# One slot sooner for key grams and norm, eight slots from 12 for the inverse's steps, and a small weight product in four parts

## What is computed

```python
for t in range(S):                                   # per batch and head: delta-rule attention
    y[:, :, t] = q[t] @ state
    state = state + beta[t] * outer(k_n[t], v[t] - k_n[t] @ state)   # k_n: k over its norm
x  = y.transpose(0, 2, 1, 3).reshape(3072, 384)
h  = x @ w_in
x2 = maximum(0.01 * h, h) @ w_out
logits = x2 @ w_gate + modality_bias[modality_id]
e = argmax(logits); gate = softmax(logits)[e]
out = gate * (maximum(x2 @ w1[e], 0) @ w2[e])        # one expert for each token
```

## Time and profile before

| what | us |
|---|---|
| median of 3 runs | 1021.66 (1021.15 to 1023.77) |
| the profiled execution's own time | 1023.64 |
| its span, first to last instruction | 1021.9 |
| PE busy (matmuls) | 932.1, 91% of the span |
| DVE busy | 554.3, 54% |
| ACT busy | 351.7, 34% |
| POOL busy | 87.8, 9% |
| mean granted clock of PE | 0.951 of full speed |

### The profile page before, as it was taken

One profiled execution on the slowest core, in us unless ns is written; L12 is line 12 of the kernel. 1 busy time (PEld: TensorE's weight loads), 2 busy tenths in 40 slices (PEclk: granted clock), 3 DMA queues, 4 the chain that ended last, 5 costly groups with the idle time before them and its releaser, 6 DMA issues.

```text
span 1021.9 us, 26857 instructions
## 1 busy us (share of the span) xinstructions
PE 932.1 (91%) x10524; PEld 832.1 (81%) x10525; DVE 554.3 (54%) x1577; ACT 351.7 (34%) x608; POOL 87.8 (9%) x100
## 2 busy tenths in 40 slices
PE   4897699999999999999999999999988999999972
PEld 4896588878888889888888888888877898888962
DVE  5936795389626983498428862334562333333341
ACT  4255234542534343433444242332511222212230
POOL 1000000000020000100010001001021212212211
PEclk8659899999999999999999999999998999999996
DMA  9803181235223440345143411317132111111122
GB/s 161 283 2 73 36 159 57 72 87 88 56 47 89 95 80 26 87 103 94 26 87 81 86 30 29 98 38 202 40 112 99 46 31 46 38 39 46 31 78 70
DMA packets 147923, 77.91 MB, mean 76 GB/s; under 512 B 112112, under 2 KB 143856, under 8 KB 147440
## 3 DMA queue, kind: packets, MB, share of 16 engines
q1 hardware_dynamic: 143728, 66.98, 27.9%
q0 software_dynamic: 4096, 9.48, 3.0%
HBM read 59.30 MB, written 13.21 MB: 71 GB/s over the span
## 4 chain that ended last, share of the span: by engine, by line
PE 73%; DVE 12%; DMA 4%; ACT 3%; issue 3%; SPq 3%; DVEq 0%; POOL 0%; ACTq 0%; POOLq 0%
PE bank L486 16%; PE bank L471 14%; PE bank L567 10%; PE bank L542 9%; PE bank L430 3%; PE bank L457 2%; PE bank L415 2%; PE bank L454 2%; PE bank L362 2%; SPq L737 2%; PE bank L552 2%; DVE inv_t L1264 2%; DVE inv_tmp L1258 2%; PE bank L504 2%; PE bank L383 1%
## 5 line engine op out<-in xcount | busy, mean ns | idle before, releaser
L486 PE MATMUL bank<-wo_hi,g_hi 128*128 128x392 f32 x384 | 138.8, 361 | 8.3 <-DVE g_lo L1338 5.4
L1011 ACT ACTIVATE g_raw<-bank 128x512 f32<-128x512 f32 x96 | 57.3, 597 | 227.4 <-PE bank L471 225.0
L1333 DVE SCALAR_TENSOR_TENSOR g_raw<-g_raw 128x512 f32<-128x512 f32 x96 | 66.2, 690 | 123.6 <-ACT g_raw L1011 122.8
L471 PE MATMUL bank<-x_hi,wi_hi 128*128 128x512 f32 x288 | 118.2, 411 | 16.1 <-DVE x_lo L1329 12.6
L486 PE MATMUL bank<-wo_hi,g_lo 128*128 128x392 f32 x384 | 132.0, 344 | 0.0
L486 PE MATMUL bank<-wo_lo,g_hi 128*128 128x392 f32 x384 | 131.8, 343 | 0.0
L471 PE MATMUL bank<-x_hi,wi_lo 128*128 128x512 f32 x288 | 113.7, 395 | 0.0
L471 PE MATMUL bank<-x_lo,wi_hi 128*128 128x512 f32 x288 | 113.6, 394 | 0.0
L1018 ACT ACTIVATE g_hi<-g_raw 128x512 fp32r<-128x512 f32 x96 | 60.6, 631 | 105.7 <-DVE g_raw L1333 102.6
L1338 DVE TENSOR_TENSOR g_lo<-g_raw,g_hi 128x512 fp32r<-128x512 f32 x96 | 66.1, 689 | 41.8 <-ACT g_hi L1018 40.9
L486 PEld LDWEIGHTS bank<-wo_hi,g_hi 128*128 128x128 f32 x384 | 72.7, 189 | 14.2 <-issue 6.8
(11 more groups left out here) (211 smaller groups left out, 1664.2 us busy)
## 6 DMA issues: line engine op xcount, KB each, us to landing
wo_lo<-wo_lo_d SPq DMA_DIRECT2D x80, 196.0 KB
w_raw<-in_moe_w SPq DMA_DIRECT2D x6, 1536.0 KB, 8.4
x_rows<-stage SPq DMA_DIRECT2D x6, 770.0 KB
kq_in_rows<-in_k SPq DMA_DIRECT2D x6, 768.0 KB, 5.4
k_raw<-in_k SPq DMA_DIRECT2D x24, 192.0 KB, 4.6
vals<-in_v SPq DMA_DIRECT2D x24, 192.0 KB, 4.7
kq_in_rows<-in_q SPq DMA_DIRECT2D x6, 768.0 KB, 7.8
x_raw<-y_t SPq DMA_DIRECT2D x36, 96.0 KB, 2.5
```

The costliest lines, as they stand in the source:

```text
L471: mm = pe.matmul(bank[0][:], a[:, m, P * f:P * f + P], x[:, m, :], start=(m == 0 and x is x_hi and a is wi_hi), stop=(m == KT - 1 and a is ...
L486: mm = pe.matmul(acc[i][:, 0:DX], g[f % 2][:, P * i:P * i + P], w, start=(f == 0 and k == 0), stop=(f == FT - 1 and k == 2))
L1011: act.activation(g_raw[f % 2][:], bank[0][:], ACT.Copy).then_inc(s.hs_ev, 1)
L1333: dve.scalar_tensor_tensor(out=g_raw[f % 2][:], in0=g_raw[f % 2][:], scalar=0.01, in1=g_raw[f % 2][:], op0=ALU.mult, op1=ALU.max).then_inc ...
```

## The change

The table gives the steps of the inverse to eight slots from 12 on, where it gave them to eight from 13 on. The key grams (`gram_k`, their copies, `norm`, `roots`, `scale_gram`) stand a slot sooner in every set, and all four `keys_t` in slot 8. `gate_weights` is cut at slices 9, 11 and 14: nine slices stay in slot (-1, 4), two go to slot 11, three to slot 12 between the two parts of `state_sum`, two to slot 13 ahead of `up(0, 0)`. The tiles `wo_t` move off x_raw to a place that `no_token` also holds, so ACT waits for the end of `clear_list`'s transfer ahead of its first copy; SP's wait ahead of `load_x(0)` goes.

```diff
-INV_AT = {13: (0, 5), 14: (5, 9), 15: (9, 13), 0: (13, 17), 1: (17, 21), 2: (21, 25), 3: (25, 30), 4: (30, INV)}
+INV_AT = {12: (0, 4), 13: (4, 8), 14: (8, 11), 15: (11, 15), 0: (15, 19), 1: (19, 23), 2: (23, 27), 3: (27, INV)}
...
-        wo_t = [same_place(f"wo_t{i}", [P, KT, P], sb.at + 4 * DM * i, F32) for i in range(2)]
+        wo_t = [same_place(f"wo_t{i}", [P, KT, P], sb.at + at, F32) for i, at in enumerate((2560, 6144))]
...                                       # PE
+                    gate_weights(14, FT)
                     up(0, 0)
...
-                    if f == 10:
-                        gram_k(n + 2, 0)
-                    if f == 11:
-                        gram_k(n + 2, 2)
...
                 if n == -1 and f == 4:
-                    gate_weights()
+                    gate_weights(0, 9)
+                if n == -1 and f == 11:
+                    gate_weights(9, 11)
+                if n == -1 and f == 12:
+                    gate_weights(11, 14)
...
                     if f == 8:
-                        keys_t(n + 2, 0)
-                        keys_t(n + 2, 1)
+                        for m in range(4):
+                            keys_t(n + 2, m)
                     if f == 9:
-                        keys_t(n + 2, 2)
-                        keys_t(n + 2, 3)
+                        gram_k(n + 2, 0)
+                        gram_k(n + 2, 1)
                     if f == 10:
-                        gram_k(n + 2, 1)
-                    if f == 11:
+                        gram_k(n + 2, 2)
                         gram_k(n + 2, 3)
...                                       # SP
-                if n == -1 and f == 10:
-                    sp.wait_ge(s.wx_mm, FT)
...                                       # ACT
+            def gate_weights(first, end):
+                if first == 0:
+                    act.wait_ge(s.list_out, 16)
+                for f in range(first, end):
...
-                    if f == 12:
                         roots(n + 2)
...
+                if n == -1 and f == 11:
+                    gate_weights(9, 11)
                 if n == -1 and f == 12:
+                    gate_weights(11, 14)
                     split_x(0)
...                                       # DVE
-                if nxt and f == 13:
+                if nxt and f == 12:
                     scale_gram(n + 2)
...
-                    if f == 12:
                         norm(n + 2)
```

More of the change, by code:

```diff
@@ L488, in down @@
                 mm.then_inc(s.l2_mm, 1)
[L490 to L493, removed]
+            def gate_weights(first, end):
+                if first == 0:
+                    pe.wait_ge(s.misc_in, 16 * 6)
+                for f in range(first, end + 1):
+                    if f < end:
                         if f % 4 == 0:
@@ L500, in gate_weights @@
                         mm.then_inc(s.wt_mm, 1)
-                    if f:
+                    if f > first:
                         pe.wait_ge(s.wt_ev, f)
@@ L1025, in copy_acc, with gate_weights @@
                     act.activation(stage[:, i, :], acc[i][:, 0:DX], ACT.Copy).then_inc(s.acc_ev, 1)
-            def gate_weights():
-                for f in range(FT):
+            def gate_weights(first, end):
+                if first == 0:
+                    act.wait_ge(s.list_out, 16)
+                for f in range(first, end):
                     act.wait_ge(s.wt_mm, f + 1)
@@ L1032, in gate_weights, with gate_columns @@
                     act.activation(wo_t[f % 2][:].rearrange("p a b -> p (a b)"), bank[2 + f % 3][:, 0:DM], ACT.Copy).then_inc(s.wt_ev, 1)
+            def gate_columns():
                 act.wait_ge(s.wx_mm, FT)
@@ L1062, in slot @@
                 if n == -1 and f == 13:
+                    gate_weights(14, FT)
+                    gate_columns()
                     small_h(0, 0)
@@ L1102, in slot @@
                     if f == 8:
-                        copy_t(k_t, "KT", n + 2, 0)
-                        copy_t(k_t, "KT", n + 2, 1)
+                        for m in range(4):
+                            copy_t(k_t, "KT", n + 2, m)
                     if f == 9:
-                        copy_t(k_t, "KT", n + 2, 2)
-                        copy_t(k_t, "KT", n + 2, 3)
+                        copy_gram(n + 2, 0)
                     if f == 10:
-                        copy_gram(n + 2, 0)
+                        copy_gram(n + 2, 2)
                     if f == 11:
-                        copy_gram(n + 2, 2)
-                    if f == 12:
                         roots(n + 2)
@@ L1506, in slot @@
                     split_x(0)
+                    rest_gate_weights()
                     leaky(0, 0)
                     rest_g(0, 0)
-                inv = range(*INV_AT[f]) if f in INV_AT and (nxt if f >= 13 else cur) else range(0)
-                inv_set = n + 2 if f >= 13 else n + 1
-                if nxt and f == 13:
+                inv = range(*INV_AT[f]) if f in INV_AT and (nxt if f >= 12 else cur) else range(0)
+                inv_set = n + 2 if f >= 12 else n + 1
+                if nxt and f == 12:
                     scale_gram(n + 2)
@@ L1540, in slot @@
                 if nxt:
+                    if f == 9:
+                        copy_gram(n + 2, 1)
                     if f == 10:
-                        copy_gram(n + 2, 1)
+                        copy_gram(n + 2, 3)
                     if f == 11:
-                        copy_gram(n + 2, 3)
-                    if f == 12:
                         norm(n + 2)
@@ L1561, in slot @@
                 if n == -1 and f == 5:
-                    rest_gate_weights()
                     token_biases()
```

## The result

The changed kernel took 1025.66 us (median; 1024.03 to 1027.08), the kernel before on the same chip 1021.66. The ratio is 1.0045 with an interval of 1.0023 to 1.0066: slower by 4.6 us (the medians are 4.0 apart), where 1.1 less was forecast. The median is 1.4 above the upper end of the range. The profiled execution took 1025.3, with a span of 1023.5. That is only 1.6 above the span before; the rest of the difference does not show between these two traces.

The account below looks back on a forecast made before the run. It took the small product, then DVE's chain, to bound the ramp, and PE the rest; 4.0 us later at `up(0, 0)` less 1.5, 0.8, 1.2 and 1.6 gave -1.1, so 1021.66 became 1020.6 us, range 1014.0 to 1024.3.

Parts of the forecast that it names:

- Step 1: Slot (-1, 4): ACT's first copy waits for the list until 43.3, `merge_x` starts at 59.3, 5.6 us sooner; 4.5 taken as gained.
- Steps 2 and 3: Ramp, slots 8 to 13: norm's transpose one us sooner, product slices delay `up(0, 0)` by 8.5 us, 4.0 net, to 110.3.
- Steps 4 to 6: Behind `up(0, 0)`: -1.5 at `split_wo(0)`, -0.8 at `tr`, -1.2 at x_lo of block 1, -1.6 at `tr` in four other blocks.
- The sum of -1.1: Whole kernel: 4.0 - 1.5 - 0.8 - 1.2 - 1.6 = -1.1 us, span 1021.9 to 1020.8.
- step 6: Sets 2 to 5: shorter waits of `merge_x` for `tr`, 4 x 0.4 = -1.6 us; moved pieces in slots 8 to 13 cost nothing.
- rival 3: Slots 8 to 10: bunched transposes and grams wait for banks, four sets x 0.5, +2.0 us, 1022.6; chance 0.14.
- the prediction's own signs of being wrong: `up(0, 0)` starting before 107 or after 112.5, or new PE waits in slots 8 to 10 of blocks 0 to 3.
- Rival 1: Slots 11 to 13 of the ramp: product slices run at full clock, 6.4 us less, 1014.2; chance 0.22.
- rival 2: Behind `up(0, 0)`: clock stays low through `down(0, 0)` and `up(0, 2)`, +4.2 us, 1024.8; chance 0.12.
- Rival 4: Slot (-1, 4): list lands at 48.9 us or later, so the 4.5 us are lost, 1025.1; chance 0.04.

Follow-up runs that it names:

- no_list: Changed kernel with `wo_t` where `no_token` does not reach, so ACT's first copy does not wait for `clear_list`'s transfer; 1012.69 us, ratio 0.9957 to the kernel before.
- copy_ahead: Changed kernel with ACT's copies of slices 9 and 10 put ahead of `roots` in slot 11; 1014.63 us, ratio 0.9934 to the kernel before.
- rest_behind: Changed kernel with slices 9 to 15 of the product in one piece in slot 13, behind both halves of `state_sum`; 1018.13 us, ratio 0.9999 to the kernel before.
- gate_alone2: Kernel before with only the product in four parts and `wo_t` moved, run once more; 1026.74 us, ratio 1.0069, no pauses.
- before_trace3: Kernel before, unchanged, third trace; `up(0, 0)` at 105.9 us, no pauses.
- after_third: Changed kernel, unaltered, run a third time on another chip; 1019.73 us, ratio 0.9988 to the kernel before, no pauses.
- after_fourth: Changed kernel, unaltered, run a fourth time; 1021.64 us, ratio 0.9998 to the kernel before, no pauses.
- set 2: Kernels measured together on another chip: the kernel before (1019.35 us), no_list, rest_behind, and the changed kernel with key grams singly (1019.02 us).
- before_trace4: Kernel before, unchanged, fourth trace; `up(0, 0)` at 103.1 us, two small pauses.
- grams_alone: Kernel before with only grams and norm a slot sooner and the table from 12; 1026.2 us, ratio 1.0049; once more in a set without pauses: 1020.1 us, 1.0003.
- gate_alone: Kernel before with only the product in four parts and `wo_t` moved, first run; 1027.12 us, ratio 1.0067, with pauses.
- set 1: Kernels measured together on another chip: changed kernel again (1026.9 us), gate_alone, grams_alone, and the changed kernel with the old table (1030.56 us).

## Why the prediction was wrong, step by step

**Step 1, the first part of the product, was right.** 43.20 for 43.3, 59.10 for 59.3. no_list shows it causally: the list's landing moves `merge_x` and `up(0, 0)` one to one.

**Steps 2 and 3, the chain to `up(0, 0)`, had the mechanism right, and the number with luck:** 110.30 for 110.3, with the clock at 0.50 all through. The norm's transpose started at 91.98, 1.5 sooner than worked out (98.0 - 4.5 = 93.5). Most of that is step 1's gain, which came whole: the clock rose 5.5 sooner, and `old_values` began at 72.35 for 78.00, 5.65 sooner and not 4.5. From there PE's five pieces took 15.7 in place of 14.1, so that the two errors cancel. copy_ahead and rest_behind confirm the two causes, ACT's roots ahead of the copies and the slices themselves. gate_alone2 has the same sign: this half of the change costs 5.2 us at the start and gives nothing back.

**Steps 4 to 6, what DVE gives back, were right term by term.** At `up(0, 7)` the 3.96 by which the changed kernel was late have shrunk to 1.02, by 2.9 where 1.5 + 0.8 was forecast. `merge_x` gains 0.45 in each of four blocks, 1.8 for 1.6. x_lo of block 1 gained 0.5 in this trace, of the 1.2 forecast. The sum of -1.1 is not shown by this. Against before_trace3, a trace without pauses and with the same long start (span 1018.1), the two traces of the changed kernel without pauses stand 1.8 below (after_third, 1016.3) and 2.5 above (after_fourth, 1020.6). Of the -1.8, 1.3 is a shorter wait for `ht_lo` among the experts, which the change does not touch (5.9 for 7.2); of the +2.5, one further low stretch is some 1.6. At `up(4, 0)`, where the sum had -0.7, the two were 0.3 and 1.2 behind, the second with that further stretch in it.

**What failed is the carrying of the sum to the median, and the nothing that step 6 put for the moved grams in slots 8 to 13, with rival 3's price for it.** Two things were missing. For the first the evidence is four traces, so it is argued more than shown.

First, the sum was held against one trace, and its difference of -1.1 was then taken off the median. The kernel before has two starts, 3.0 us apart, and the trace at hand had the long one; its own time stood 2.0 above the median, which the prediction named and passed over. Against the short start the sum of -1.1 would be +1.9. In four traces the changed kernel had only one start. How often the kernel before takes the short one is not measured; two of four traces did. If it is half, this is worth 1.5, an estimate. It may be more: the 35 runs before of set 2 reach from 1006.9 to 1025.0, and before_trace4, with the short start, took 1014.2, so there are faster courses than those traced.

Second, step 6 said that PE shows no wait in slots 8 to 13, and rival 3 named the right slots with the wrong mechanism and price. It looked for waits for banks, 4 x 0.5, at 0.14. There are none. But these slots carry pauses that no engine causes, already to be seen in the trace of before (2.4 us at L457), and with the grams in pairs they come to 2.5 us more. New waits in these slots were also one of the prediction's own signs of being wrong. I read past a wait under "issue" in the very slots into which the change moves work. In a set without pauses slots 9 to 13 lose 0.1 to 0.2 per block, and that is all.

With the -1.8 and the +2.5 above as ends, these give an estimate of +2.2 to +6.5 for the set of the result (-1.8 + 1.5 + 2.5 and 2.5 + 1.5 + 2.5), around the 4.6 measured; without pauses -0.3 to +4.0, where -1.2 and -0.2 were measured. Two traces can't place it better. The medians say that the pauses go with more than the 2.5 that the traces show: from the sets with pauses to those without, the ratio of the changed kernel falls by 4.8 to 6.3 us and that of grams_alone by 4.7, while that of gate_alone, which has the old order of the grams, stays (1.0067 and 1.0069). Each ratio has an interval of some 2.5 us to either side, so what is above 2.5 is not clear of noise. It stays open what the pauses are, why one chip or hour has them and another not, and whether grams one by one avoid them: none of the three sets that had them showed a pause.

**The rivals.** Rival 1 (full clock in slots 11 to 13) and rival 2 (low clock behind `up(0, 0)`) fell with the two windows above, 0.50 and then 1.00. Rival 4 fell with the landing at 43.2. What the Trainium skill states in "TensorE: Matmul & The Clock Gate", "What's actually happening", that sustained activity of PE brings the full clock, the traces bear out no better than before: PE was busy for 18.27 of 20.30 us at 0.50.

## What to carry to other kernels

A profiled execution is one draw: when its time is off the median by more than the effect that is forecast, look for the place where executions differ before carrying a difference over, and forecast against each start. A wait under "issue" in slots into which small matmuls are moved can grow with them, so it needs a price in the sum. A variant that is level in one place can pay in another: the grams one by one left slots 9 to 13 as they were and cost 1.2 us at x_lo of block 1. And when work is spread into gaps of PE, follow it on the queue of the engine that must drain it: here two copies of ACT, queued behind a wait for DVE's norm, cost 3.7 us at the first product, and one place ahead in the same queue took 0.5% off the time.

## What the runs showed of the hardware

- PE can pause for 0.2 to 1.1 us in a dense row of small matmuls without any releaser in the trace. The first trace of the kernel before, the first of the changed one and all four of set 1 had it, in slots 10 and 11 of the blocks; of the other fourteen traces thirteen had none there and one had two of 0.3.
- The granted clock came up for one stretch of 3.4 us amid the small product in two of four traces of the same kernel and stayed at 0.50 in the other two. PE was busy for all of the 3.3 us ahead of it in three of them, and for 3.25 in the fourth, one of those in which it came up. These 3.4 us at full clock brought `up(0, 0)` 3 us ahead.
- A matmul product 8 columns wide, with the transposes that go with it, kept PE busy without a break for 15.4 us (the changed kernel) to 29.6 us (the first trace of the kernel before) at 0.50, and for 15.4 us or more in each of the twenty traces.
